# Reordering zeros, means' loads, a value sum and block maxima at the start of an attention and mixture-of-experts kernel

## The reference

```python
# attention: q, k, v are (2, 8, 768, 64) float32
k_sum = k.reshape(B, H, nb, 32, D).max(axis=3)      # block maxima of k
v_sum = v.reshape(B, H, nb, 32, D).mean(axis=3)     # block means of v
scores_l = where(|i - j| < 16, scale * q @ k.T, -1e9)
scores_s = scale * q @ k_sum.T + log(32)
a = softmax(concat([scores_l, scores_s]))
attn = a @ concat([v, v_sum])
# mixture of experts over the 1536 rows x of attn (512 wide), 8 experts, top 1
logits = normed(x) @ normed(expert_emb).T / tau
out[mask_e] = gate[mask_e] * (relu(x[mask_e] @ w1[e]) @ w2[e])
# a last MLP, 512 -> 2048 -> 512, with a rational function between
h = x @ w_in;  g = P(h) / (Q(h) + 1e-6);  y = g @ w_out
```

## Time and profile before

| what | before |
|---|---|
| median of 3 runs | 713.1 us |
| the three runs | 707.41 to 714.42 us |
| the profiled execution | 710.13 us |
| its span, first to last instruction | 708.6 us |
| mean granted TensorE clock of it | 0.98 |

### The profile page before, as it was taken

The page is one execution under the profiler, slowest core; times in us unless marked ns, Lnnn a source line. Parts: engine busy times, 40 slices in busy tenths (PEclk is TensorE's granted clock), DMA queues, the critical chain, the costliest instruction groups (busy, mean ns, idle before and its releaser), DMA issues.

```text
span 708.6 us, 11258 instructions
## 1 busy us (share of the span) xinstructions
PE 676.5 (95%) x3326; PEld 539.2 (76%) x3326; DVE 491.1 (69%) x981; ACT 409.8 (58%) x774; POOL 162.3 (23%) x213
## 2 busy tenths in 40 slices
PE   5889889999779999999999999999999999999997
PEld 5567667777668778888888888888888888888885
DVE  6856636766747798313323447999989899898886
ACT  7545536564446677433434446876666666676664
POOL 3449599621411002230100300101011000020000
PEclk9979979999989999999999999999999999999999
DMA  8679879741975799328413610100001000010001
GB/s 298 151 191 275 218 196 221 167 110 50 320 282 211 275 361 376 103 47 275 172 46 97 223 68 31 45 1 30 16 16 59 1 16 0 1 60 1 1 0 59
DMA packets 57906, 89.80 MB, mean 127 GB/s; under 512 B 32352, under 2 KB 32368, under 8 KB 56696
## 3 DMA queue, kind: packets, MB, share of 16 engines
q1 hardware_dynamic: 49880, 64.91, 30.2%
q0 software_dynamic: 7520, 24.15, 10.5%
q10 hardware_dynamic: 448, 0.02, 0.1%
HBM read 63.50 MB, written 16.63 MB: 113 GB/s over the span
## 4 chain that ended last, share of the span: by engine, by line
PE 84%; DMA 6%; DVE 3%; ACT 2%; POOL 1%; issue 1%; SPq 1%; ACTq 0%; POOLq 0%; DVEq 0%
PE bank L1779 19%; PE bank L1794 18%; PE bank L1742 13%; PE bank L1721 13%; PE bank L1512 9%; PE bank L1607 4%; PE bank L1581 3%; PE bank L1606 3%; PE bank L1624 2%; DMA x_by_slot<-x_all 1%; DMA kraw<-in_k_dram 1%; DMA raw_late<-in_moe_w_dram 1%; DMA xg<-x_by_slot 1%; PE bank L1526 1%; DVE weights L1259 1%
## 5 line engine op out<-in xcount | busy, mean ns | idle before, releaser
L1779 PE MATMUL bank<-X2T,weights 128*128 128x512 f32 x576 | 143.1, 398 | 0.0
L1794 PE MATMUL bank<-weights,G 128*128 128x512 f32 x576 | 139.4, 391 | 1.8 <-DVE G L1259 1.8
L1794 PEld LDWEIGHTS bank<-weights,G 128*128 128x128 f32 x576 | 108.1, 188 | 26.3 <-DVE G L1259 2.6
L1779 PEld LDWEIGHTS bank<-X2T,weights 128*128 128x128 f32 x576 | 107.8, 188 | 24.8
L1742 PE MATMUL bank<-weights,HT 128*128 (+1 forms) x456 | 113.3, 404 | 1.1 <-DVE HT L1259 1.1
L1721 PE MATMUL bank<-weights,XT 128*128 (+1 forms) x432 | 108.7, 401 | 3.4 <-DVE weights L1259 2.7
L1742 PEld LDWEIGHTS bank<-weights,HT 128*128 128x128 f32 x456 | 85.9, 192 | 20.9 <-issue 1.3
L1721 PEld LDWEIGHTS bank<-weights,XT 128*128 128x128 f32 x432 | 79.7, 188 | 22.9 <-issue 4.3
L933 ACT ACTIVATE qd<-bank,coef 128x512 f32<-128x512 f32 x48 | 33.1, 689 | 75.9 <-PE bank L1779 75.7
L830 ACT ACTIVATE es<-es,nmx 128x182 f32<-128x182 f32 x96 | 42.5, 443 | 58.1 <-DVE nmx L1127 57.9
L1259 DVE TENSOR_TENSOR HT<-bank,HT 128x512 fp32r<-128x512 f32 x38 | 24.4, 685 | 62.4 <-ACT HT L961 62.4
(11 more groups left out here) (244 smaller groups left out, 1136.7 us busy)
## 6 DMA issues: line engine op xcount, KB each, us to landing
raw_early<-in_moe_w_dram SPq DMA_DIRECT2D x14, 1024.0 KB, 6.4
raw_late<-in_moe_w_dram SPq DMA_DIRECT2D x14, 1024.0 KB, 8.7
KWs<-KW SPq DMA_DIRECT2D x48, 182.0 KB, 4.5
y_in_order<-yo POOLq DMA_DIRECT2D x19, 256.0 KB
xg<-x_by_slot POOLq DMA_DIRECT2D x18, 256.0 KB, 6.1
x_all<-in_moe_w_dram POOLq DMA_DIRECT2D x8, 512.0 KB, 6.4
qraw<-in_q_dram SPq DMA_DIRECT2D x12, 256.0 KB, 5.1
VA<-in_v_dram SPq DMA_DIRECT2D x10, 208.0 KB
```

The costliest lines, as they stand in the source:

```text
L1779: last = T_.matmul(bank[6 + f % 2][:, :], W[:, 0, wa, kc * F2 + f * P:kc * F2 + (f + 1) * P], X2T[c % 2][:, xa, kc * C_TOK:(kc + 1) * C_TO ...
L1794: last = T_.matmul(bank[tt][:, :], G[:, f % 2, ga, tt * P:(tt + 1) * P], W[:, 1, wa, f * DM:(f + 1) * DM], start=(f == 0 and n_ == 0), sto ...
```

## The change

Four moves in the orders of SP, GpSimd, VectorE and TensorE. No instruction is added or taken away, and no wait is changed.

- SP: `load_means(0)`, `(1)` go ahead of tile 1's exchanges. `zero_part(0)` follows `load_v_all(2)`; `zero_part(1)` and `(2)` go ahead of `load_v(2)` and `load_v(3)`.
- GpSimd: `mean_v(2)` goes ahead of the first two weight requests.
- VectorE: `place_embedding` goes ahead of `key_max(0)`.
- TensorE: `key_maxima(1)` goes between the second and third matmul of `value_sums(1)`.

```diff
             store_means(0)
             store_means(1)
+            load_means(0)
+            load_means(1)
             swap_windows(1, 0)
             swap_windows(1, 1)
-            load_means(0)
-            load_means(1)
             load_q(3)
             load_v_all(2)
+            zero_part(0)
             for T in range(2, NT):
                 swap_windows(T, 0)
                 swap_windows(T, 1)
                 if T + 2 < NT:
                     load_q(T + 2)
+                if 0 < T - 1 < ZERO_PARTS:
+                    zero_part(T - 1)
                 load_v(T)
-                if T < 2 + ZERO_PARTS:
-                    zero_part(T - 2)
...
+            mean_v(2)
             load_raw(0)
             load_raw(1)
-            mean_v(2)
...
             key_lo(1)
+            place_embedding()
             key_max(0, ROW // 2)
-            place_embedding()
             key_max(1, ROW // 2)
...
-            def value_sums(g):
+            def value_sums(g, first, last):
                 pe.wait_ge(v_all_in[g], 16)
-                for j in range(4):
-                    last = T_.matmul(bank[(7, KT_BANKS)[g]][:, :], ident[:, :], vraw[g][:, j * BANK:(j + 1) * BANK],
+                for j in range(first, last):
+                    sum_ = T_.matmul(bank[(7, KT_BANKS)[g]][:, :], ident[:, :], vraw[g][:, j * BANK:(j + 1) * BANK],
                                      start=(j == 0), stop=(j == 3))
-                last.then_inc(vm_mm, 1)
+                if last == 4:
+                    sum_.then_inc(vm_mm, 1)
...
-            value_sums(0)
-            value_sums(1)
+            value_sums(0, 0, 4)
+            value_sums(1, 0, 2)
             key_maxima(1)
+            value_sums(1, 2, 4)
```

## The result

| | before | after |
|---|---|---|
| median of 20 runs each | 709.1 us | 703.2 us |
| range | 699.4 to 719.4 us | 699.1 to 711.6 us |
| profiled execution, span | 708.6 us | 698.6 us |

The ratio of after to before is 0.9942, with a 95% interval of 0.9918 to 0.9966: faster, by 0.6%, where 13.3 us or 1.9% had been forecast. That ratio shows less than the medians' 0.9917 because the ratios here leave out runs more than 1.5% above the fastest of their kernel; their number differs from chip to chip, so across chips only medians are compared. The 703.2 us lie inside the range given, yet the change was 5.9 us by the medians and 0.6% by the ratio, less than half of what was forecast. The forecast had also set the kernel before at 713.1, from three runs; twenty put it at 709.1.

A forecast was written before the change was run, and what follows sets the result against it. TensorE, with 84% of the span, was taken as the bound. The stall's 9.3 us plus tile 5 earlier (86.5 - 82.5) gave 13.3: 710.1 - 13.3 = 696.8, with the median's 3.0 699.8 us; range 693.5 to 706.8.

The forecast's parts named there:

- The stall and its price: Ahead of tile 5's scores, the scatter's wait for zeros costs 9.3 us: about 5 waiting, the rest at lower clock.
- Block maxima, VectorE's order: Early in attention, moving `key_maxima(1)` brings the first windows 1.7 us earlier; moving `place_embedding` is worth 0.
- Means' loads ahead of exchanges: On SP, the means' loads go out 0 to 0.8 us earlier, 0.7 taken; tile 1 loses 1 us.
- Third value sum: On GpSimd, `mean_v(2)` starts at 44.5; work up to the scatter begins 5.3 us earlier and grows by 2.
- Scatter to tile 5: From GpSimd's scatter to tile 5's scores takes 5.7 us, so tile 5 can start at 80.8, or 84.7 if delayed.
- The gain of clock in the early stretch: Near 39 us, a shorter wait for the means may keep the clock up, worth up to 5.1 us.
- The new wait with a new slow stretch: Rival, 0.18: tile 3, 4 or 5 waits for its exchange and the clock falls; gain 8.2, 704.9 us.
- the exchanges of tile 2 come late: Rival, 0.06: behind the zeros, tile 2's exchange lands 7.7 to 9.5 us later; gain 6.3, 706.8 us.
- a shorter gap would not be enough: Near 39 us the clock falls anyway: early gain 3.2 us, whole gain 12.5 instead of 13.3.

The follow-up runs named there:

- e9: The kernel before with 22 matmuls of the identity on itself in the wait ahead of tile 5's first scores: 706.8 us beside 710.8, ratio 0.9948.
- e1: The kernel before with only the three zero parts moved on SP: 700.9 us beside 709.5, ratio 0.9910.
- e8: The changed kernel with both means' loads and third value sum back in their old places: 698.9 us beside 710.8, ratio 0.9833.
- e5: The changed kernel with the means' loads behind tile 1's exchanges again: 698.8 us beside 710.1, ratio 0.9848.
- e13: The changed kernel with the means' loads behind tile 1's exchanges, run a second time: 697.2 us beside 709.4, ratio 0.9857.
- e12: The changed kernel unaltered, measured a third time: 705.0 us beside 709.4 for the kernel before, ratio 0.9971.
- e0: The changed kernel unaltered, measured again: 702.7 us beside 709.5 for the kernel before, ratio 0.9918.
- e6: The kernel before with 44 matmuls of the identity on itself in the wait ahead of tile 5's first scores: ratio 1.000.
- e2: The changed kernel with the zeros left in their old places: 708.8 us beside 709.5 for the kernel before, ratio 1.0039.
- e4: The changed kernel with the third value sum behind the two weight requests again: 702.7 us beside 710.1, ratio 0.9896.

## Why the prediction was wrong

**The stall and its price: right.** It was 9.3 us, half wait and half clock. e9 took the clock's half alone (4.0 us), and e1, the zeros alone, took 8.6 us in the medians.

**Block maxima, VectorE's order: right.** The first windows started at 25.64, 1.4 us earlier (forecast 1.7), the first product at 36.10, and `key_max(2)` cost 0.6 us where half was set against it. No run makes this edit alone or parts VectorE's move from TensorE's; e8, which adds both to e1's zeros, gained 11.9 us in the medians against e1's 8.6, on another chip.

**Means' loads ahead of exchanges: the step that failed.** The prediction counted 0.7 us for the move, looked for its price "on tile 1" and found 1 us there. It did not ask what else stands behind the waiting load on SP: q of tile 3 and the group 2 values, on which GpSimd waits. The first product gained 0.2 us. The issue of the values came 1.4 us later than without the move and the transfer then took 3 us more; this edit turned a gain of 11 to 12 us (e5, e13) into 4 to 7 (e12, after, e0). That those 11 to 12 us lie near the forecast 13.3 is partly luck, as the terms below were too large.

**Third value sum: sized wrong.** "Its values had landed at 44.3" carried the 7.7 us over to a kernel in which the means' place made the transfer longer. They landed 10.0 us after issue, at 46.1, so that GpSimd's block of sum and requests began 3.6 us earlier and not 5.3. And e1 starts the sum at 46.28 with no move at all, since TensorE without its slow stretch near 39 us frees the requests early. No run shows a worth of the edit by itself.

**Scatter to tile 5: sized wrong.** The 5.7 us of before were measured with DMA engines that were half idle, a share of 0.54 from 85.66 to 91.40. After, from 75.83 to 85.68, it was 9.85 us at a share of 1.03, with weights and values under way (e13 shows the same, 9.44 us); tile 5 started at 85.7, not 82.5. This bound, 84.7 at the latest in the text, was passed.

**The gain of clock in the early stretch (5.1 us): sized too high.** It rested on one execution in which a 1.87 us wait was followed by a fall. Four profiled executions have this wait, of 1.68 to 1.87 us: a fall follows in two, of 10.2 us (before) and 6.8 us (e6), and none in the other two (e1, e9). In the typical run little is left of it: e1, with the wait, has a median of 11.2 us at the lower clock, e5 and e13, with one of 0.97 and 0.63 us, have 9.1 and 9.7.

**The rivals.** The new wait with a new slow stretch (8.2 us forecast) was nearest for the typical run: three waits of 1.1 to 1.7 us, and 17 us at the lower clock in the median where the profile shows 7. That the exchanges of tile 2 come late happened as well, at 1.1 us; it needed the zeros and the early means together, as neither e2 nor e13 shows it. In the fourteen profiles whose first product waited 1.1 us or less no fall came near 39 us. By the rule of the Trainium skill (TensorE: Matmul & The Clock Gate, Part 1) that the throttled state is the default and activity releases it, the prediction had feared that a shorter gap would not be enough; at this place the traces do not bear that out, while e4's 1.75 us at tile 3 shows that a wait no longer than the old one can still be followed by a fall.

## What to carry to other kernels

Where a DMA issue must wait for an earlier one to land, look at every issue behind it in that queue and at the engine that waits for the last of them; put issues that are ready ahead of it. Take the time of a transfer from a stretch as crowded as the one it moves to. And where runs differ by more than the effect, read the time at the lower clock of many runs before a single profile is taken for the typical one.

## What the hardware showed unexpectedly

- The same wait of 1.9 us was followed by 10 us at 1.2 GHz in one execution (before) and by none in another (e1). A stall of 4.9 us went with 10 us of it, one of 5.5 us (e2) with 20, and one of 1.75 us (e4) with 20 too, though in that execution one of 2.03 us had gone with none.
- One kernel's time at the lower clock ranged from 11 to 45 us over 92 runs, and with it the span from 697 to 718 us.
- The same 1 MB load took 6.6 us when issued at 34.7 (e13) and 9.8 us when issued at 36.2 (e12), in kernels that differ in the place of two 48 KB loads alone. One MB of zeros issued right behind it did not lengthen it (6.8 us in e1, 10.9 without them in e2).
